# Expert rows as 128 + 96 with four 32-column matmuls side by side, in place of 112 + 112

## The reference, cut to what matters

```python
def _moe2_ref(x, w_gate, w1, w2):
    N, D = x.shape                 # 1792, 768
    E = w_gate.shape[1]            # 8 experts, inner size 1024
    cap = N // E                   # 224 rows each
    ...                            # greedy: every expert gets exactly cap rows
    for e in range(E):
        mask = assigned == e
        h = np.maximum(x[mask] @ w1[e], 0.0)
        out[mask] = h @ w2[e]
    return out
```

## Time and profile before

| | us |
|---|---|
| median of 3 runs | 1069.16 (1068.51 to 1069.37) |
| the profiled execution | 1069.24 |
| its span | 1067.3 |
| mean granted TensorE clock | 0.989 of full |
| first product of expert 0 begins | 810.46 |
| second product of expert 7 begins | 1043.51 |

### The profile page before, as it was taken

The page is one execution under the profiler, slowest core; times in us unless marked ns, Lnnn a source line. Parts: engine busy times, 40 slices in busy tenths (PEclk is TensorE's granted clock), DMA queues, the critical chain, the costliest instruction groups (busy, mean ns, idle before and its releaser), DMA issues.

```text
span 1067.3 us, 23613 instructions
## 1 busy us (share of the span) xinstructions
PE 1030.2 (97%) x8724; PEld 752.5 (71%) x8724; DVE 819.7 (77%) x1699; ACT 588.9 (55%) x942; POOL 197.3 (18%) x319
## 2 busy tenths in 40 slices
PE   6999999999999999999999999999987999999996
PEld 3444444444469999999976666666656889888895
DVE  5899999999968656665686667666678899999971
ACT  5888888989846233333461111313215688877791
POOL 3444444444310000000000000000001132212211
PEclk9999999999999999999999999999997999999998
DMA  3752211121033000000241040401048566677401
GB/s 93 206 143 60 65 55 52 52 60 52 19 128 119 2 1 2 2 2 1 89 150 31 16 149 16 149 16 31 16 148 276 181 234 233 248 269 286 158 14 52
DMA packets 66782, 103.44 MB, mean 97 GB/s; under 512 B 14480, under 2 KB 44432, under 8 KB 66704
## 3 DMA queue, kind: packets, MB, share of 16 engines
q1 hardware_dynamic: 64144, 91.34, 26.0%
q0 software_dynamic: 2560, 11.01, 3.4%
HBM read 91.32 MB, written 11.01 MB: 96 GB/s over the span
## 4 chain that ended last, share of the span: by engine, by line
PE 84%; DVE 9%; issue 4%; ACT 1%; DMA 1%; POOL 0%; SPq 0%; DVEq 0%; POOLq 0%; ACTq 0%
PE psum L1465 21%; PE psum L1652 17%; PE psum L1760 10%; PE psum L1746 9%; PE psum L1510 6%; PE psum L1495 6%; PE psum L1519 5%; PE psum L1655 3%; DVE arena L1030 2%; PE psum L1685 2%; PE psum L1542 1%; PE psum L1728 1%; PE psum L1581 1%; DVE arena L1364 1%; DVE arena L1354 1%
## 5 line engine op out<-in xcount | busy, mean ns | idle before, releaser
L1465 PE MATMUL psum<-arena 128*128 128x224 f16 x2304 | 224.4, 259 | 1.6 <-DVE arena L1002 1.0
L1465 PEld LDWEIGHTS psum<-arena 128*128 128x128 f16 x2304 | 219.8, 98 | 6.1 <-issue 3.2
L1652 PE MATMUL psum<-arena 128*128 128x384 f16 x1152 | 195.9, 326 | 0.0
L1652 PEld LDWEIGHTS psum<-arena 128*128 128x128 f16 x1152 | 107.7, 98 | 66.8 <-issue 0.8
L590 POOL TENSOR_SCALAR arena<-arena 128x448 f32<-128x448 f32 x168 | 105.5, 639 | 160.9 <-DVE arena L1012 160.9
L1760 PE MATMUL psum<-arena 128*112 128x384 f16 x768 | 127.1, 326 | 0.4 <-issue 0.4
L723 ACT ACTIVATE arena<-arena 128x448 f32<-128x448 f32 x168 | 125.6, 750 | 1.0 <-DVE arena L1032 1.0
L805 ACT ACTIVATE arena<-psum,arena 128x384 f32<-128x384 f32 x28 | 16.3, 581 | 186.5 <-PE psum L1652 144.3
L1746 PE MATMUL psum<-arena 128*128 128x224 f16 x1152 | 114.5, 262 | 3.8 <-DVE arena L1390 2.0
L1760 PEld LDWEIGHTS psum<-arena 128*112 128x112 f16 x768 | 99.3, 130 | 24.8 <-issue 0.8
L1746 PEld LDWEIGHTS psum<-arena 128*128 128x128 f16 x1152 | 111.9, 99 | 6.2 <-DVE arena L1390 2.4
(11 more groups left out here) (238 smaller groups left out, 1389.4 us busy)
## 6 DMA issues: line engine op xcount, KB each, us to landing
arena<-moe_w SPq DMA_DIRECT2D x16, 3072.0 KB, 11.7
arena<-moe_w_out SPq DMA_DIRECT2D x32, 384.0 KB, 3.9
arena<-moe_w_in SPq DMA_DIRECT2D x16, 384.0 KB, 4.5
arena<-q SPq DMA_DIRECT2D x24, 224.0 KB, 2.7
arena<-v SPq DMA_DIRECT2D x24, 192.0 KB, 2.4
arena<-k SPq DMA_DIRECT2D x24, 96.0 KB, 2.6
arena<-k SPq DMA_DIRECT2D x48, 48.0 KB, 2.3
y_rows<-arena SPq DMA_DIRECT2D x4, 336.0 KB, 2.4
```

The source lines that it names most:

```text
L1465: last = pe.matmul(out, w_split[:, f, z, k * 128:(k + 1) * 128], x[u % 2][:, k, :], start=(k == 0 and m == 0), stop=(k == KD - 1 and m == 2))
L1652: last = pe.matmul(psum[:, BANK_Y + q % 4, 0:HALF], g_pair(p)[:, x, k, i * 128:(i + 1) * 128], w_split[:, k, z, columns], **flags)
```

## The change

Each expert's 224 rows are split into 128 and 96. The one-hot table of the rank has 128 columns, the first gather and the first column of ids carry 128 rows, the second 96, and so do the scatters. In the second product, jobs 2 and 3 are now the 128 rows, a half of the output columns each, 24 matmuls with 128 stationary columns. Jobs 0 and 1 are the 96 rows, in groups of four matmuls with 32 stationary columns that write four different sets of 32 PSUM partitions. Job 0 has 24 such groups: rows 0 to 31 and 32 to 63 of the 96, each for both halves of the columns. Job 1 has 12: rows 64 to 95 for both halves, each as two partial sums of twelve terms in different partitions. ScalarE copies job 0 by two instructions. Of job 1 it copies the first partial sums by two, and VectorE adds the second partial sums to them, by two `scalar_tensor_tensor` instructions (`rows_sum`). In steps 0 to 5 this stands in `up_lo` between the second and the third quarter of the first weights; in step 6 behind `w2_scale`, ahead of all of step 7; in step 7 behind `rows_scale`. The second increment of the output semaphore `s_o` for an expert thus comes after VectorE's sum, and job 3 waits for it, since it writes the same bank; GpSimd scatters the 96 rows after it. `group_hot` also moves to other words. The diff, without the edits that only replace `TP` by `FULL` in the router and in tile declarations:

```diff
...
@@ -52,6 +52,8 @@
 MAIN = 3 * WIDE
 NKEY = 3
 QK_ROWS = (TP, 128)
+FULL = 128
+SLOTS = (FULL, CAP - FULL)
 BEHIND = 2
 BLK = 32
 NB = DM // BLK
...
@@ -641,14 +644,14 @@
 
             def gather_rows(e):
                 hold(s_tT, 3 * e)
-                pool.tensor_copy(row_idx[0:TP], ids[0:TP, bass.ds(2 * e, 2)]).then_inc(s_gidx, 1)
+                pool.tensor_copy(row_idx, ids[:, bass.ds(2 * e, 2)]).then_inc(s_gidx, 1)
                 hold(s_gidx, e + 1)
                 if first(e):
                     for t in range(NTILE - 4, NTILE):
                         hold(s_yw[t % 4], y_written(t))
                 for c in range(2):
-                    pool.indirect_dma_start(out=yg[0:TP, c, :], out_offset=None, in_=y_d[:, :],
-                                            in_offset=bass.IndirectOffsetOnAxis(ap=row_idx[0:TP, c:c + 1], axis=0)).then_inc(s_ygl[c], 16)
+                    pool.indirect_dma_start(out=yg[0:SLOTS[c], c, :], out_offset=None, in_=y_d[:, :],
+                                            in_offset=bass.IndirectOffsetOnAxis(ap=row_idx[0:SLOTS[c], c:c + 1], axis=0)).then_inc(s_ygl[c], 16)
 
             def step(e):
                 if expert_live(e + 2):
...
@@ -666,13 +669,13 @@
                     else:
                         pool.partition_all_reduce(eh_amax, eh_max, 128, RMAX).then_inc(s_ea, 1)
                 if expert_live(e):
-                    pool.tensor_copy(idx[0:TP], ids[0:TP, bass.ds(2 * e, 2)]).then_inc(s_idx, 1)
+                    pool.tensor_copy(idx, ids[:, bass.ds(2 * e, 2)]).then_inc(s_idx, 1)
                     hold(s_idx, e + 1)
-                for c in range(2):
+                for j, c in ((1, 1), (3, 0)):
                     if expert_live(e):
-                        hold(s_o, 4 * e + 2 * c + 4)
-                        pool.indirect_dma_start(out=out_d, out_offset=bass.IndirectOffsetOnAxis(ap=idx[0:TP, c:c + 1], axis=0),
-                                                in_=e_out[0:TP, c, :], in_offset=None).then_inc(s_sct, 16)
+                        hold(s_o, 4 * e + j + 3)
+                        pool.indirect_dma_start(out=out_d, out_offset=bass.IndirectOffsetOnAxis(ap=idx[0:SLOTS[c], c:c + 1], axis=0),
+                                                in_=e_out[0:SLOTS[c], c, :], in_offset=None).then_inc(s_sct, 16)
                 if expert_live(e):
                     hold(s_sct, 32 * (e + 1))
                     pool.sem_inc(s_free, 1)
...
@@ -905,8 +908,17 @@
                         wait(act, s_E2, 4 * e + j + 2)
                         wait(act, s_oi, e + 1)
                         wait(act, s_free, e + 1)
-                        act.activation(e_out[0:TP, j // 2, (j % 2) * (DM // 2):(j % 2 + 1) * (DM // 2)],
-                                       psum[0:TP, BANK_E2 + j % 2, 0:DM // 2], ACT.Copy, scale=o_inv[0:TP]).then_inc(s_o, 1)
+                        if j == 2:
+                            wait(act, s_o, 4 * e + 4)
+                        source = psum[:, BANK_E2 + j % 2, 0:HALF]
+                        if j >= 2:
+                            act.activation(e_out[:, 0, (j % 2) * HALF:(j % 2 + 1) * HALF], source, ACT.Copy, scale=o_inv).then_inc(s_o, 1)
+                            return
+                        rows = slice(0, 64) if j == 0 else slice(64, 96)
+                        for n in range(2):
+                            part = slice(64 * n, 64 * n + 64 - 32 * j)
+                            last = act.activation(e_out[rows, 1, n * HALF:(n + 1) * HALF], source[part], ACT.Copy, scale=o_inv[part])
+                        last.then_inc(s_o if j == 0 else s_op, 1)
 
                 rows_out(0)
                 if is_last(e + 1):
...
@@ -1331,18 +1343,18 @@
             emit(dve.tensor_reduce(rank[0:TP], place[0:TP], AX.X, ALU.add))
             link(dve.tensor_tensor(newly[0:TP], held[0:TP], over_chunks(e2[0:TP]), ALU.mult))
             emit(dve.tensor_reduce(pair_of[0:TP], newly[0:TP], AX.X, ALU.add))
-            link(dve.tensor_scalar(half_of[0:TP], rank[0:TP], float(TP), None, ALU.is_ge))
+            link(dve.tensor_scalar(half_of[0:TP], rank[0:TP], float(FULL), None, ALU.is_ge))
             emit(dve.tensor_tensor(group_of[0:TP], pair_of[0:TP], half_of[0:TP], ALU.add))
-            link(dve.scalar_tensor_tensor(low_of[0:TP], half_of[0:TP], -float(TP), rank[0:TP], ALU.mult, ALU.add))
+            link(dve.scalar_tensor_tensor(low_of[0:TP], half_of[0:TP], -float(FULL), rank[0:TP], ALU.mult, ALU.add))
             link(dve.tensor_tensor(group_hot[0:TP], group_of[0:TP].unsqueeze(2).broadcast_to([TP, CH, CH]),
                                    groups[0:TP].unsqueeze(1).broadcast_to([TP, CH, CH]), ALU.is_equal))
             dve.tensor_tensor(group_tok[0:TP], group_hot[0:TP], tok[0:TP].unsqueeze(2).broadcast_to([TP, CH, CH]), ALU.mult).then_inc(s_hot, 1)
             for h in range(2):
                 half = slice(h * CH // 2, (h + 1) * CH // 2)
-                dve.tensor_tensor(low_hot[0:TP, half], low_of[0:TP, half].unsqueeze(2).broadcast_to([TP, CH // 2, TP]),
-                                  lows[0:TP].unsqueeze(1).broadcast_to([TP, CH // 2, TP]), ALU.is_equal).then_inc(s_hot, 1)
+                dve.tensor_tensor(low_hot[0:TP, half], low_of[0:TP, half].unsqueeze(2).broadcast_to([TP, CH // 2, FULL]),
+                                  lows[0:TP].unsqueeze(1).broadcast_to([TP, CH // 2, FULL]), ALU.is_equal).then_inc(s_hot, 1)
             dve.wait_ge(s_idm, 1)
-            dve.tensor_copy(ids[0:TP], psum[0:TP, BANK_IDS, 0:CH]).then_inc(s_ids, 1)
+            dve.tensor_copy(ids, psum[:, BANK_IDS, 0:CH]).then_inc(s_ids, 1)
             dve.wait_ge(s_exta, 2)
             link(dve.tensor_reduce(ym, y_top, AX.X, ALU.max))
             pow2_scale(dve, ym, y2_inv, y2_scl, s_rc, total[0])
...
@@ -1375,8 +1387,17 @@
                     wait(dve, s_we2, W2_STEPS * e + 1)
                     pow2_scale(dve, w2_amax, w2_inv, w2_scl, s_we2, W2_STEPS * e + 1)
 
+                def rows_sum(e):
+                    wait(dve, s_op, e + 1)
+                    for n in range(2):
+                        part, rows = slice(64 * n + 32, 64 * n + 64), e_out[64:96, 1, n * HALF:(n + 1) * HALF]
+                        last = dve.scalar_tensor_tensor(rows, psum[part, BANK_E2 + 1, 0:HALF], o_inv[part], rows, ALU.mult, ALU.add)
+                    last.then_inc(s_o, 1)
+
                 def up_lo(e):
                     for j in range(3):
+                        if j == 2 and expert_live(e - 2):
+                            rows_sum(e - 2)
                         w1_lo(e, j)
                     if first(e):
                         w1_lo(e, 3)
...
@@ -1410,6 +1431,7 @@
                         w2_lo(e, j)
                 if is_last(e):
                     rows_scale(e)
+                    rows_sum(e)
                 if expert_live(e + 2):
                     if not first(e + 2):
                         w_absmax(e + 2, 0, s_w1l, w1_max, s_wm1)
...
@@ -1449,6 +1471,8 @@
                 if expert_live(e + 1):
                     if not first(e + 1):
                         w2_scale(e + 1)
+                    if is_last(e + 1):
+                        rows_sum(e)
                     if not is_last(e + 1):
                         rows_scale(e + 1)
             expert_steps(dve, step)
...
@@ -1725,8 +1749,8 @@
                 for c in range(2):
                     wait(pe, s_ygl[c], 16 * (e + 1))
                     for k in range(KD):
-                        last = pe.transpose(psum[:, BANK_ET + k // 2, (k % 2) * CAP + c * TP:(k % 2) * CAP + (c + 1) * TP],
-                                            yg[0:TP, c, k * 128:(k + 1) * 128], ident[0:TP, 0:TP])
+                        n, base = SLOTS[c], (k % 2) * CAP + c * FULL
+                        last = pe.transpose(psum[:, BANK_ET + k // 2, base:base + n], yg[0:n, c, k * 128:(k + 1) * 128], ident[0:n, 0:n])
                         if c == 1 and k % 2 == 1:
                             last.then_inc(s_tT, 1)
 
...
@@ -1748,17 +1772,26 @@
                     last.then_inc(s_E1, 1)
 
             def expert_down(e, j):
-                c, half = j // 2, j % 2
                 wait(pe, s_eL, 2 * (e + 1))
                 wait(pe, s_w2L, 4 * (e + 1))
                 wait(pe, s_o, 4 * e + j + 1)
+                pe.sem_inc(s_pe, 1)
                 hh, hl = (x.rearrange("p (k t) -> p k t", k=KE) for x in eh_parts(e))
                 wH, wL = (w.rearrange("p (k n) -> p k n", k=KE) for w in w2_parts(e))
-                for k in range(KE):
-                    cols = slice(half * (DM // 2), (half + 1) * (DM // 2))
-                    for m, (h, w) in enumerate(((hh, wH), (hh, wL), (hl, wH))):
-                        last = pe.matmul(psum[0:TP, BANK_E2 + j % 2, 0:DM // 2], h[:, k, c * TP:(c + 1) * TP], w[:, k, cols],
-                                         start=(k == 0 and m == 0), stop=(k == KE - 1 and m == 2))
```

(26 more changed lines are left out.)

3 lines of the change are left out of this document (1 added, 2 removed).

## The result

The changed kernel takes 1087.15 us (median of four), the kernel before 1069.26 in the same measurement. The ratio is 1.0168, with a 95% interval of 1.0156 to 1.0181: slower by 18 us, where 13 were forecast, inside the range of 1074 to 1092.

What follows compares the result with a forecast made beforehand. TensorE bounds a step at 30.55 us, VectorE second, 0.8 us behind. The terms 0.4 + 6.1 + 5.75 + 2.75 - 1.95 + 0.3 = 13.35 us give 1082.6 us (chance 0.50), range 1074 to 1092.

Steps and rivals of the forecast that it cites:

- part 2: VectorE's sum in each expert: two added instructions cost 1.1 us on its own loop of 29.8 us.
- The steady step: One expert step in the middle of the run: 31.0 us against 30.55 before, slower by 0.45 us.
- part 3: Place of the sum: job 3 waits for it on a shared bank, TensorE idle 2.25 us, both loops 31.0 us.
- part 4: Step 0: TensorE idles 4.5 us, the clock falls for 2.75 us; next first product +4.25 us, VectorE's next start +3.5.
- B: Rival: clock falls in the 2.25-us gaps of steps 1 to 6 too; 1086.6 us with two falls, 1094 with all; chance 0.23.
- A: Rival: the clock holds in both long gaps, step 0 and the tail: 1077.4 us; chance 0.14 together with E.
- E: Rival: bank waits as forecast, but the clock holds and the sum costs 0.3 us: 1072.6 us; chance 0.14 with A.
- part 6: Last two steps: step 6's sum waits for ScalarE, last second product starts 5.75 us later; long TensorE gap adds 2.75.
- Part 7: Small terms: wider one-hot tables 0.3 us and first gather 0.1, together +0.4; last scatter of 128 rows +0.3.
- Part 1: Second product's matmuls: groups of four cost 162.5 ns, 1.95 us less for each expert, TensorE's step 28.6 us.
- C: Rival: 32-column blocks overlap less; 1084.1 us at 205 ns a group, over 1180 without overlap; chance 0.05.
- D: Rival: VectorE has room if the sum's pair costs under 0.78 us a step: 1063.7 us, faster; chance 0.05.

Runs made afterwards that it cites:

- a bank of its own: Changed kernel with job 1 in a separate PSUM bank, so job 3 no longer waits for VectorE's sum: 1081.89 us, ratio 1.0117 to the kernel before.
- The filled gaps: Changed kernel with TensorE's idle gaps filled by matmuls whose results nobody reads: 1079.73 us, ratio 1.0105 to the kernel before.
- the reordering: Changed kernel with ScalarE's copy of expert 6's job 1 and VectorE's sum moved ahead in the last two steps: 1081.66 us, ratio 1.0114 to the kernel before.
- by columns: Changed kernel's split and 32-column groups, but the groups share the 96 rows by output columns, without partial sums: 1066.47 us, ratio 0.9973 to the kernel before.
- the kernel with the shortened loop: Kernel dividing by output columns, with VectorE's maximum of the activations moved ahead of a wait for GpSimd: 1065.11 us, ratio 0.9960 to the kernel before.

## Why the prediction was right, and what it sized wrong

**The second bound (part 2)** was right and decided the sign: VectorE 0.8 us behind TensorE, 1.3 us of sum added. Without the sum 30.05 us, with it 31.4 to 31.5, both shown alone. The sum took 1.25 us and 0.14 to release TensorE where I took 1.1; the line through two rows with 128 partitions was 12% short, and VectorE's loop grew by 1.5 us, not 1.1.

**The steady step** was forecast at 31.0 us and is 31.5. Besides the sum it is the branch at the end of VectorE's loop, 0.33 us: before, it lay under the wait for ScalarE, and I removed the wait and forgot what it covered. This is 2.4 us over five steps.

**The place of the sum (part 3)**: idle 2.25 us forecast, 2.42 to 2.59 measured, released by the sum, as said. I had both loops at 31.0 us; with a bank of its own the step is as long, so it is VectorE's loop that sets it, and the wait matters through the clock.

**Step 0 (part 4)**: idle 4.5 us forecast, 4.52 measured, with the fall. (The 1.6 us between the engines' starts in part 4 mixes two views of the profile; in one view it is the 1.8 of part 3.) The fall cost 1.7 us (5.74 against 4.06) and not 2.75, because the clock rose again sooner than behind the first gather. The first row of the table came out 1.3 us under the forecast for this and for luck: the first product of expert 0 ran less long at the low clock (its 72 matmuls took 8.45 us, before 9.73), which I had not forecast, while the one-hot tables began 0.9 us later in shared code.

**The clock in short gaps** was the term that failed, with the steady step. I took that it holds at 2.25 us (with B, that it falls, as the rival). It fell in steps 1, 3 and 6. In steps 1 and 3 it cost 1.8 us each (33.3 and 33.2 us against 31.5), 3.6 us; in step 6 it cost nothing, since the last second product waits there for VectorE's low halves, which do not wait for job 3. The five steps are so 6.35 us over the forecast: 3.6 from the clock, 2.4 from the longer step, 0.4 since five steps of 31.0 us are 2.25 us more than before and I had added 1.85. The other rows take 1.5 of that back, which leaves the whole miss of 4.85 us of span. That the sum came within 5 us is in part luck: errors of both signs cancel, and B with its two falls gave 1086.6, nearer to the 1087.15 than my case. In the expert steps the clock was at 1.2 GHz in five places and not in two: behind the gaps of steps 0, 1, 3 and 6 and in the last one. With that A and E fall. The stretches of steps 1 and 2, with the granted clock third from the end:

```profile
889.00:891.80 2.80, 0.21 (x2) 0.02 (x1) 2.72 (x4) 2.78 (x3) 0.00 (x0) 1.00 1.02 405
892.40:892.80 0.40, 0.40 (x5) 0.21 (x3) 0.40 (x1) 0.07 (x1) 0.24 (x1) 1.00 0.97 389
892.80:893.20 0.40, 0.40 (x3) 0.23 (x2) 0.40 (x1) 0.00 (x0) 0.40 (x1) 0.56 0.55 215
893.20:895.60 2.40, 2.40 (x10) 1.08 (x8) 2.37 (x3) 0.00 (x0) 1.13 (x1) 0.50 0.45 137
...
922.40:924.90 2.50, 0.12 (x1) 0.00 (x0) 2.42 (x4) 2.48 (x3) 0.00 (x0) 1.00 1.02 406
924.90:928.80 3.90, 3.86 (x24) 2.37 (x25) 3.87 (x3) 0.87 (x2) 1.78 (x1) 1.00 0.68 244
```

Through the gap of 2.6 us of step 1 the clock stays at 2.4 GHz. Job 3 begins at 891.81 at full clock, and 1.0 us into it the clock falls to 1.2 GHz (0.50), until 896.2. After the gap of 2.4 us of step 2 it does not fall. The filled gaps show that the gap is the cause, though the fall comes behind it.

**The last two steps (part 6)** were right by place and size: +5.75 forecast, +6.11 measured, and the reordering gives 4.8 us of it back. TensorE's gap there was 3.3 us, not 5.4, mostly since job 3 itself ran slow; the last product lost 2.8 us (8.85 against 6.03), 2.75 forecast.

**Part 7**: the tables cost 0.3 us as forecast (2.35 us for 2.08). The 0.3 us of the last scatter did not show: behind TensorE's end the span is 0.42 us shorter.

**Part 1** was right for the second product, 1.8 us less for each expert with 1.95 forecast. A step of TensorE's work fell by only 1.7 us, to 28.9 where I had 28.6: the first product takes 13.89 us for 13.80 and the transposes 1.21 for 1.15. C fell. D fell by the sum alone: 1.3 us is above the 0.78 that it allowed. By the Trainium skill, "TensorE: Matmul & The Clock Gate", "Measured speedup vs the span model", three such blocks gain 2.38 times, 0.79 for each block; here four gained 3.9 times (4 x 162.5 / 165.6), 0.98 for each, and the measurement decides. The Trainium skill, "TensorEngine Tiling (Array Packing)", "PSUM Bottleneck", says that tiling does not speed up emptying PSUM. The trace agrees: the copies on ScalarE went from four to six, with 1.16 to 1.17 us for a pair of the new ones against 0.58 for a full one. But that the change must be slower by this, as the prediction says, does not follow: by columns ScalarE makes seven copies and the kernel is faster. Two instructions of VectorE, 2% of its step each, turned a gain into a loss.

## What to carry to other kernels

Before making the leading engine faster, strip the second engine's step of the waits that the leader causes: what is left is the floor, and here it let through 0.5 us of the 1.7 won. Price everything that moves to that engine against this slack and not against zero, with the branches and waits that the old cover hid. Then look at the drain of the pipeline by itself, since the place of one sum cost as much there, for one expert (the 4.8 us that the new order gives back), as the slower loop did over five steps at full clock (4.6 us); and prefer to divide work by output columns where a division by terms needs a sum afterwards.

## What the runs showed of the hardware beyond expectation

- Matmuls with 32 stationary columns in four column groups came at 83 ns for four of 192 moving columns, 21 ns each, and 165.6 ns for four of 384. The gate's 30 ns is no floor.
- The granted clock can fall behind a gap of TensorE of 2.5 us, when the matmuls have begun again: it was 1.00 through the gap of step 1 and fell 1.0 us into job 3. The length of the gap does not decide it. In the run with the new order at the end two gaps of 2.53 us stand in steps 3 and 4: after the one job 3 took 4.06 us, after the other 5.74. Repeats of one kernel can so differ by some 1.7 us a fall.
- A pair of VectorE instructions of another shape between two long ones cost more than it was busy: 1.4 us for 1.15, and 1.5 for 1.25 in the changed kernel.
- In the kernel by columns TensorE paused 2.36 us in the middle of job 1 in step 1 with nothing that the profile shows as releaser, and the clock was low behind it. It cost about 3 us in that step (33.04 against 30.03). A like pause stands in job 1 of step 0 (2.13 us), and both are there in the kernel with the shortened loop (1.53 and 2.12 us), but none in steps 2 to 5, which pass through the loop's code again, nor in step 6. The loading of instructions at a first pass would fit steps 0 and 1; no run tried it, and the cause stays open.
